# Both routings' opening VectorE operations written at the end of the block ahead of each, the single-overflow branch last, and two clears given to ScalarE

## The reference, cut to what matters

```python
x = attention(q, k, v)                  # banded, 8 heads; 4 batches of 768 tokens
# first mixture: top-1 of 8 experts, no capacity limit
do_compute = (x @ w_skip) > 0
logits = x[do_compute] @ w_gate         # [N, 8]
e_idx = np.argmax(logits, axis=1)
gate_w = softmax(logits)[e_idx]
x[do_compute] += gate_w * (relu(x @ w1[e_idx]) @ w2[e_idx])
# second mixture: every expert takes exactly N / 8 = 384 tokens
order = np.argsort(-(x @ w_gate2).flatten())
for idx in order:                       # greedy, best pair of token and expert first
    tok, e = idx // 8, idx % 8
    if assigned[tok] < 0 and counts[e] < 384: assigned[tok] = e; counts[e] += 1
out[t] = relu(x[t] @ w1[assigned[t]]) @ w2[assigned[t]]
```

## Time and profile before

| | |
|---|---|
| median of 3 runs | 813.74 us (812.87 to 814.51) |
| the profiled execution | 815.21 us, of which its span is 813.5 us |
| mean granted TensorE clock | 0.970 |
| TensorE busy | 753.9 us, 93% of the span |
| VectorE, ScalarE, GpSimd busy | 66%, 56%, 20% |

### The profile page before, as it was taken

How to read it: one execution, slowest core, us unless ns; L and a number is a source line. 1 busy time by engine, 2 the same in 40 slices (tenths; PEclk the granted TensorE clock), 3 DMA queues, 4 the chain that set the end, 5 groups by cost and what they waited for, 6 DMA issues and landing times. The chain is left out here.

```text
span 813.5 us, 15742 instructions
## 1 busy us (share of the span) xinstructions
PE 753.9 (93%) x5590; PEld 675.1 (83%) x5590; DVE 537.1 (66%) x1463; ACT 453.7 (56%) x919; POOL 165.4 (20%) x184
## 2 busy tenths in 40 slices
PE   2899999999959999999999938999999999999997
PEld 2899999999928988899888825888888888888896
DVE  6877778777477778766666557766666767675420
ACT  3889888888525454554545303545554554536360
POOL 8100000000030222222221101141414141423321
PEclk9999999999959999999999957999999999999999
DMA  8998987986264666535763006768675777769861
GB/s 179 217 215 221 240 204 210 212 209 167 99 205 156 215 241 216 182 121 218 245 223 126 13 9 227 186 223 199 198 199 194 196 208 187 220 178 302 226 130 44
DMA packets 64106, 151.65 MB, mean 186 GB/s; under 512 B 12294, under 2 KB 15750, under 8 KB 64016
## 3 DMA queue, kind: packets, MB, share of 16 engines
q1 hardware_dynamic: 52512, 114.77, 48.3%
q0 software_dynamic: 11504, 35.72, 18.1%
HBM read 118.84 MB, written 16.67 MB: 167 GB/s over the span
## 5 line engine op out<-in xcount | busy, mean ns | idle before, releaser
L1817 PE MATMUL r_ph<-r_xh,r_w1h 128*128 128x384 f32 x256 | 90.6, 354 | 0.0
L1817 PE MATMUL r_ph<-r_xh,r_w1l 128*128 128x384 f32 x256 | 86.2, 337 | 0.0
L1817 PE MATMUL r_ph<-r_xl,r_w1h 128*128 128x384 f32 x256 | 85.8, 335 | 0.0
L592 ACT ACTIVATE pr<-pr,nmx 128x232 f32<-128x232 f32 (+1 forms) x192 | 79.9, 467 | 9.6 <-DVE nmx L685 9.6
L1098 PE MATMUL m_ph<-m_xh,m_w1h 128*128 128x224 f32 x288 | 80.9, 281 | 0.1
L1252 ACT ACTIVATE m_hh<-m_ph 128x224 fp32r<-128x224 f32 (+1 forms) x72 | 25.2, 350 | 97.9 <-PE m_ph L1098 93.9
L1098 PE MATMUL m_ph<-m_xh,m_w1l 128*128 128x224 f32 x288 | 79.1, 275 | 0.0
L1098 PE MATMUL m_ph<-m_xl,m_w1h 128*128 128x224 f32 x288 | 78.9, 274 | 0.0
L685 DVE CUSTOM_DVE_ANT_0 pr<-sc,bias 128x232 f32<-128x232 f32 (+1 forms) x192 | 65.0, 374 | 19.5 <-PE sc L466 17.5
L599 ACT ACTIVATE prt<-tp 128x384 f32<-128x384 f32 (+1 forms) x128 | 65.5, 537 | 22.0 <-PE tp L478 18.5
L1831 PE MATMUL r_py<-r_w2h,r_hh 128*128 128x512 f32 x192 | 76.1, 396 | 0.0
(11 more groups left out here) (298 smaller groups left out, 1960.5 us busy)
## 6 DMA issues: line engine op xcount, KB each, us to landing
r_w<-moe_w SPq DMA_DIRECT2D x64, 512.0 KB, 5.1
m_w<-moe_w SPq DMA_DIRECT2D x36, 512.0 KB, 5.9
row_buf<-moe_w SPq DMA_DIRECT2D x9, 2048.0 KB, 8.7
r_w2l<-r_w POOLq DMA_DIRECT2D x32, 512.0 KB, 4.9
k_raw<-kI SPq DMA_DIRECT2D x64, 208.0 KB, 7.2
q_raw<-qT SPq DMA_DIRECT2D x64, 192.0 KB, 7.6
vo<-vL SPq DMA_DIRECT2D x16, 384.0 KB
x_rows<-row_buf SPq DMA_DIRECT2D x4, 1536.0 KB, 6.6
```

The costliest lines, as they stand in the source:

```text
L592: nc.scalar.activation(pr[n % PRS][:, t, lo:CW], pr[n % PRS][:, t, lo:CW], ACT.Exp, bias=nmx[n % PRS][:, t:t + 1], scale=-1.0).then_inc(ex ...
L1817: last = nc.tensor.matmul(ph[m % 4][:, 0:CAP], w[:, c, m * P:(m + 1) * P], x[:, c, :], start=(c == 0 and a == 0), stop=(c == KC - 1 and a ...
```

## The change

Three edits:

1. `open_route`, a new function, holds the first seven operations of `route`. It is called at the end of VectorE's `fast` (and `general`) in the first block, on tiles made ahead of the blocks (`best1`, `work1`, `hot1` and so on). `route` begins with `expd`. The semaphore `asked` is gone; TensorE's count follows the block change directly.
2. `open_search` holds what `bests(logits2)`, `needs()` and the first lines of `attempt(0, 0)` did. It is called in the second block behind `put_z` (n = 1) or behind `keep_limits` (other n). VectorE's branches are written in another order: n = 0, n > 1, and n = 1 last.
3. The two `m_xg` clears are written by ScalarE (Copy of ones with scale 0), ahead of its first weight split, in place of GpSimd's two memsets.

```diff
@@ VectorE, end of the first block
                         for b in range(B):
                             if gate_step(2 * (4 * b + 3) + 1) + 1 == n:
                                 take_logits(b)
+                    dve.wait_ge(read, B)
+                    open_route(link)
...
+                def open_route(link):
+                    by_expert = [P, E, NT]
+                    dve.wait_ge(filled, FILLS + 3)
+                    link(v.tensor_reduce(best1[:], logits[:, :, 0:E], AX.X, ALU.max))
+                    link(v.tensor_tensor(work1[:], logits[:, :, 0:E].rearrange("p t e -> p e t"), best1[:].unsqueeze(1).broadcast_to(by_expert), ALU.is_equal))
+                    link(v.tensor_scalar(live1[:], logits[:, :, E], 0.0, None, ALU.is_gt))
+                    link(v.tensor_tensor(work1[:], work1[:], firstb1[:].unsqueeze(2).broadcast_to(by_expert), ALU.mult))
+                    link(v.tensor_reduce(bestw1[:], work1[:].rearrange("p e t -> p t e"), AX.X, ALU.max))
+                    link(v.tensor_tensor(work1[:], work1[:], bestw1[:].unsqueeze(1).broadcast_to(by_expert), ALU.is_equal))
+                    link(v.tensor_tensor(hot1[:], work1[:], live1[:].unsqueeze(1).broadcast_to(by_expert), ALU.mult))
@@ GpSimd, start of the second block
-                for s in range(2):
-                    g.memset(xg[s][:], 0.0).then_inc(cleared, 1)
                 g.memset(never[:], NO_ROW).then_inc(cleared, 1)
                 pool.wait_ge(cleared, 3)
@@ TensorE, start of the second block
-                pe.wait_ge(asked, 1)
                 flat = hot[:].rearrange("p e t -> p (e t)")
@@ ScalarE, start of the second block
+                for s in range(2):
+                    nc.scalar.activation(xg[s][:].rearrange("p t d -> p (t d)"),
+                                         ones[:, 0:1].broadcast_to([P, TT1 * DM]), ACT.Copy, scale=0.0).then_inc(cleared, 1)
                 for c in (0, 1):
                     w1_part(0, c)
@@ VectorE, end of the second block
+                def open_search(link):
+                    link(v.tensor_reduce(best2[:], logits2[:], AX.X, ALU.max))
+                    ...
+                    link(v.scalar_tensor_tensor(out=candf2[:], in0=steps_f[:, 0, :], scalar=span2[:, 0:1],
+                                                in1=bottom[:].broadcast_to([P, CANDS]), op0=ALU.mult, op1=ALU.add))
...
+                with dve.If(n < 1):
+                    limits_of_all(Chain(dve, alone_chain))
+                with dve.If(n > 1):
+                    one_block(E, P)
+                    y_keep(E, 0)
+                    z_part(E, 0, 2)
+                    with dve.Fori(1, OVER) as j:
+                        with dve.If(n > j):
+                            more(E + j)
+                    limits_of_all(Chain(dve, alone_chain))
                 with dve.If(n > 0):
-                    one_block(E, P)
                     with dve.If(n < 2):
+                        one_block(E, P)
                         alone = Chain(dve, alone_chain)
...
                         put_z(alone)
-                    with dve.If(n > 1):
-                        y_keep(E, 0)
-                        z_part(E, 0, 2)
-                further(dve, n, more)
-                for other in (n < 1, n > 1):
-                    with dve.If(other):
-                        alone = Chain(dve, alone_chain)
-                        limit(alone)
-                        limit_all(alone)
-                        keep_limits(alone)
+                        open_search(alone)
@@ VectorE, start of the third block
-                bests(logits2)
-                needs()
                 for r in range(TRIES):
                     attempt(0, r)
```

More of the change, by code:

```diff
@@ L782, in general @@
                         gate_dve(dve, b, logits, lp, G1, gsems)
+                    at(dve, gsems[3], B)
+                    open_route(Chain(dve, chain, setup_links))
                 by_path(dve, fast, general)
@@ L1374, in route @@
                 def route():
[L1376 to L1379, removed]
-                    link(v.tensor_reduce(bestw[:], work[:].rearrange("p e t -> p t e"), AX.X, ALU.max))
-                    link(v.tensor_tensor(work[:], work[:], bestw[:].unsqueeze(1).broadcast_to(by_expert), ALU.is_equal))
-                    v.tensor_tensor(hot[:], work[:], live[:].unsqueeze(1).broadcast_to(by_expert), ALU.mult).then_inc(asked, 1)
                     v.tensor_tensor(expd[:], logits[:, :, 0:E], best[:].unsqueeze(2).broadcast_to(shape), ALU.subtract).then_inc(shifted, 1)
@@ new lines, in limits_of_all, with more @@
+                def limits_of_all(alone):
+                    limit(alone)
+                    limit_all(alone)
+                    keep_limits(alone)
+                    open_search(alone)
+                def more(k):
+                    next_parts(k, 0, P)
+                    one_block(k, P)
+                    y_keep(k, 0)
+                    for i in range(3):
+                        z_part(k, 0, i)
+                with dve.If(n < 1):
+                    limits_of_all(Chain(dve, alone_chain))
@@ L1607, in build @@
             masked, tie, ranks = (tb(x, shape) for x in ("masked", "tie", "ranks"))
-            work, hot, gt, taken = (tb(x, shape, BF16) for x in ("work", "hot", "over", "taken"))
+            work, hot, best, bestm, bestw, need, needc, scr8, span, candf = (
+                work2, hot2, best2, bestm2, bestw2, need2, needc2, scr2, span2, candf2)
+            gt, taken = (tb(x, shape, BF16) for x in ("over", "taken"))
             firstb = firstb1
-            best, bestm, cmp1, rank1, high = (tb(x, [P, NT]) for x in ("best", "bestm", "cmp1", "rank1", "high"))
-            bestw, cmpb, ours, mem, upto, low = (tb(x, [P, NT], BF16) for x in ("bestw", "cmpb", "ours", "mem", "upto", "low"))
+            cmp1, rank1, high = (tb(x, [P, NT]) for x in ("cmp1", "rank1", "high"))
+            cmpb, ours, mem, upto, low = (tb(x, [P, NT], BF16) for x in ("cmpb", "ours", "mem", "upto", "low"))
             cmp_ = tb("cmp", [P, NT, RADIX], BF16)
```

58 lines of the change are left out of this document (34 added, 24 removed).

## The result

| | median | runs | against before |
|---|---|---|---|
| before, measured beside it | 814.31 us | 11 (812.87 to 814.63) | |
| changed | 811.79 us | 11 (811.26 to 812.36) | 0.9973, 95% interval 0.9964 to 0.9983 |
| changed, measured again | 811.79 us | 9 (810.54 to 811.88) | 0.9970, 0.9958 to 0.9982 |

The change wins 0.27%: some 2.2 us by the ratio, 2.5 by the medians, where the sum said 3.18. The profiled execution took 812.34 us, its span is 810.6, the mean granted clock 0.975 (before: 815.21, 813.5, 0.970). This is the page's row of busy times, which answers the earlier trace rows: the same work but for the two clears, which went from GpSimd to ScalarE, so what was won is standing still.

What follows compares the result with a forecast made beforehand. TensorE, busy 93% of the span, leaves gains only where it idles at two block changes, the first set by VectorE's chain. 0.75 + 2.43 = 3.18 us off 813.74 gives 810.56, forecast 810.6 us, range 809.3 to 812.8.

Steps and rivals of the forecast that it cites:

- the sum: Gains at the two block changes added: 0.75 + 2.43 = 3.18 us.
- First place: First block change, VectorE's chain to the scan: `live` no longer held by GpSimd's memsets, 0.75 us won, 0 to 0.89.
- the term for the block change: Each of the two block changes costs 0.73 us, as measured at the first in the kernel before.
- Second place: Second block change, `put_z` to compare L2017: ten operations moved ahead, 6.25 us becoming 3.82, 2.43 won.
- The jumps of VectorE: Four conditional jumps behind `put_z`: together 2.43 us if VectorE was last to arrive.
- What is later in exchange: First block change 2.64 us later, delaying ScalarE, GpSimd and SyncE work: hidden, price 0 for VectorE, at worst 0.9.
- the meeting that I priced: GpSimd's empty gather, ending at 235.0, overlaps VectorE's `picks`: GpSimd pays some 0.6 us, VectorE 0.
- Overflow block: Three VectorE jumps ahead of its first operation, at most 1.8 us, start slipping about 0.9: price 0.
- B: Second block change: VectorE's stillness stays as a wait for its own code, only 0.75 won, 813.0 us; chance 0.11.
- C: Second block change: TensorE's code fetched late, costing 0.4 to 0.9 us, about 811.3; chance 0.07.
- D: TensorE's clock rises later in the products behind the idle places; 10 us later gives 815.5; chance 0.04.
- E: First block change: removing GpSimd's clear does nothing, `live` is slow by itself, 811.3 us; chance 0.05.

Runs made afterwards that it cites:

- e4: Kernel before with the first routing's opening operations moved ahead of the block's end, GpSimd still clearing: 814.56 us, 1.0002 of before.
- e8: Kernel before with ScalarE clearing the rows in GpSimd's stead, nothing else: 0.9987 of before.
- e2: Kernel before with the search's first operations moved ahead of the overflow block's end, VectorE's branches in their old order: 813.93 us, 0.9993 of before.
- e1: Kernel before with VectorE's new order of branches alone, nothing moved: 813.74 us, 0.9998 of before.
- e5: Kernel before with both VectorE's and TensorE's branches in the new order, nothing moved: 819.18 us, 1.0059 of before.
- e3: Kernel before with the search's first operations moved and VectorE's new order of branches, first routing unchanged: 0.9978 of before.
- e6: Changed kernel with TensorE's single overflow block last as well: 818.63 us, 1.0055 of before.
- e7: Changed kernel with 24 more VectorE instructions in a branch not taken, moving all later VectorE code: 810.26 us, 0.9954 of before.

## Why the prediction was right, and where it was not

The time came to 811.79, inside the range and beyond 0.2% on the faster side, 1.2 us above the number. Half of that is the base: the forecast started from 813.74, the median of three executions, and the eleven beside the changed kernel gave 814.31. The other half is the gain, 2.52 by the medians instead of 3.18.

- **First place, 0.75 forecast, 0.59 found.** That `live` falls to 0.18 without the meeting was right, and L1377 was hardly slowed (0.49 beside the clearing, 0.47 without). So the 0.89 that follows from the rule of the Trainium skill (GPSIMD Engine Reference, Key points) on operations with two SBUF inputs did not come. Two things were wrong. "Moving alone is therefore worth 0" overlooked that the move takes `live` out of GpSimd's way by itself; e4 and e8 show the two edits to be worth 0.61 and 0.77 alone and 0.59 together. And the term for the block change, 0.73, was mis-sized: it measured 0.95 behind moved operations. Why it is longer there no run tells.
- **Second place, 2.43 forecast, 2.62 found** (the block change was 0.53 and not 0.73; with an earlier fall of the clock it is 2.3, see e2). I had left open who was last, and gave the sum both ways; e1 and e5 settle that it was TensorE. Its arrival sets the still time, and the ten moved operations lie in its shadow. I had it there by 473.52; with the block change at 0.53 it was 473.72, still ahead of VectorE's moved operations. The jumps of VectorE, which I had priced at up to 2.43, cost 1.1 (e2 against e3), and only with the move. The prediction calls itself wrong if the code's path, and not the work, sets when an engine may start behind a block change. In before it did so, by TensorE's path; the sum held because the moved work hides that path, not because it is gone.
- **What is later in exchange: nothing**, as said. The empty gather ended at 233.61, just before `picks`, and not at 235.0: it started at 232.31, 1.0 us after the end of ScalarE's second clear (229.33 + 2.00), where I had put 2.04. So the meeting that I priced did not happen; the real gather started at 238.22.
- **Overflow block: price 0**, right for VectorE, whose tests had cover. For TensorE the same step costs 7 us (e6 against the changed kernel: 818.63 and 811.79): the 4.2 us above, and its clock, which falls in that stillness and reads 0.50 from 452 to 456, in this windows view of e5_both_orders (columns as in the earlier trace rows):

```profile
450.00:452.00 2.00, 0.00 (x0) 0.00 (x0) 0.00 (x0) 0.00 (x0) 0.24 (x1) 0.66 0.26 75
452.00:456.00 4.00, 3.87 (x19) 3.87 (x19) 0.75 (x2) 0.80 (x2) 0.00 (x0) 0.50 0.02 4
456.00:458.00 2.00, 2.00 (x13) 2.00 (x13) 0.53 (x2) 0.79 (x2) 0.00 (x0) 0.63 0.00 0
```

- **Rivals.** B fell: 0.53 and not 3.15. C fell: TensorE's first count stands 0.61 behind the compare's start (474.06 - 473.45), as in before (477.95 - 477.34). D fell: this windows view of the changed kernel has the rise within 240 to 242, 1.6 us earlier than in before. E fell with `live`.

```profile
238.00:240.00 2.00, 2.00 (x6) 0.71 (x5) 2.00 (x3) 0.00 (x0) 1.48 (x2) 0.50 0.69 250
240.00:242.00 2.00, 2.00 (x9) 0.83 (x8) 2.00 (x3) 0.00 (x0) 1.70 (x2) 0.79 0.49 141
```

- **What the sum lacked.** The two places gave 3.21, next to 3.18. That is luck in part: the first fell short by 0.16, the second came out 0.19 better. By the traces, the miss is mostly a term that I did not have: the change also lengthens VectorE's code ahead of the search, and two edges of that code now fall where VectorE's chain is the bound, 0.6 us. The times alone can't tell this. The remaining 0.3 of the 0.88 given back (0.18 before the second expert, 0.14 at the fifth's gather) is of the size by which these intervals differ between all the runs (34.4 to 35.0 us for the first of them), and stays unexplained.

## What to carry to other kernels

Where all engines wait for each other at a block's end, find the one that comes last by what stands behind its own last operation, not by the engine whose idle row is longest; then either fill the others' wait with work, which paid here, or shorten the late engine's way, but not by putting its skipped branches ahead of work that it bounds, which cost 7 us here. Two edits that remove the same collision were worth one here: try each alone. And in a chain tuned to tenths of a microsecond, compare the chain row by row behind an edit even where nothing was edited, since moved code can cost more than a removed operation gives.

## What was not expected of the hardware

- VectorE stops for about 0.3 us at some places of its program that are, to 4 places, multiples of 128 instructions apart (0.55 instead of 0.19 us ahead of L2064; 0.24 instead of 0 at L2100). The Trainium skill (Runtime: NRT & Kernel Launch, Instruction fetch mechanics) has the code refilled in blocks of 256 instructions and the crossing of one mostly hidden. The distances of 384 in e2 and e7 do not fit 256, and two crossings of the changed kernel were not hidden.
- TensorE needs some 3 us behind its last product to pass three tests with untaken bodies and come to the next block, and 4.2 us of issue when the other branches stand ahead of the overflow block, 2.41 of them between two neighbouring products; VectorE passes its own in 1.1.
- The same gather, issued at the same time by GpSimd (606.53 and 606.55), lands in time for TensorE or 1.3 us late from one execution of the same kernel to the next.
